# Causal scores of linear attention on TensorE: products of 64 by 128 tiles split into 64 by 64 tiles, without the covered quadrant

## The reference, cut to what matters

```python
gamma = 1.0 - 2.0 ** (-5.0 - np.arange(H, dtype=np.float32))
scale = 1.0 / np.sqrt(D)
for t in range(S):
    state = gamma[None, :, None, None] * state + np.einsum('bhd,bhe->bhde', k[:, :, t], v[:, :, t])
    y[:, :, t] = scale * np.einsum('bhd,bhde->bhe', q[:, :, t], state)
...
x = np.ascontiguousarray(attn_out.transpose(0, 2, 1, 3)).reshape(B * S, H * D)
x = _moe_ref(x=x, **moe_kwargs)
return _moe2_ref(x=x, **moe2_kwargs)
```

## Time and profile before

| what | value |
| --- | --- |
| median of 3 runs | 537.28 us |
| lowest and highest | 535.38 and 537.73 us |
| the profiled execution, its own time | 538.69 us |
| its span, first to last instruction | 536.8 us |
| mean granted TensorE clock | 0.975 |
| TensorE busy | 495.5 us, 92% of the span |
| VectorE, ScalarE, GpSimd busy | 280.7, 183.0, 255.1 us |
| moved by transfers | 106.87 MB, mean 199 GB/s |

### The profile page before, as it was taken

One profiled execution on the slowest core, in us unless ns is written; L12 is line 12 of the kernel. 1 busy time (PEld: TensorE's weight loads), 2 busy tenths in 40 slices (PEclk: granted clock), 3 DMA queues, 4 the chain that ended last, 5 costly groups with the idle time before them and its releaser, 6 DMA issues.

```text
span 536.8 us, 13517 instructions
## 1 busy us (share of the span) xinstructions
PE 495.5 (92%) x4820; PEld 288.6 (54%) x4821; DVE 280.7 (52%) x467; ACT 183.0 (34%) x322; POOL 255.1 (48%) x217
## 2 busy tenths in 40 slices
PE   4999999987985777899999999999999999999995
PEld 4877777863475343444544545445445445455452
DVE  2785777676230798563646464564645333423422
ACT  0111212221002546845555463645542222223210
POOL 1222222202000013476777868787868666666553
PEclk9998999997999789999999999999999999999998
DMA  8999999998999999343366332132332432433410
GB/s 281 398 352 387 360 384 403 382 342 319 374 426 429 405 414 387 130 164 122 159 218 200 122 119 59 21 53 42 50 53 44 55 45 44 57 43 45 58 19 0
DMA packets 35095, 106.87 MB, mean 199 GB/s; under 512 B 11871, under 2 KB 13135, under 8 KB 32624
## 3 DMA queue, kind: packets, MB, share of 16 engines
q1 hardware_dynamic: 20880, 91.85, 44.4%
q0 software_dynamic: 14176, 14.49, 15.0%
HBM read 92.82 MB, written 29.43 MB: 228 GB/s over the span
## 4 chain that ended last, share of the span: by engine, by line
PE 82%; DVE 6%; issue 5%; DMA 4%; POOL 1%; ACT 1%; SPq 0%; DVEq 0%; POOLq 0%
PE ps L1017 52%; PE ps L1000 5%; PE ps L675 4%; PE ps L739 4%; DMA late_w1a<-chunks 3%; PE ps L859 3%; PE ps L888 3%; PE ps L715 2%; PE ps L729 2%; PE ps L750 2%; PE ps L689 1%; PE ps L771 1%; DMA w_region<-chunks 1%; POOL rec_region L613 1%; PE ps L704 1%
## 5 line engine op out<-in xcount | busy, mean ns | idle before, releaser
L1017 PE MATMUL ps<-w_region,s_region 128*128 (+1 forms) x1304 | 290.4, 379 | 0.3 <-issue 0.3
L1017 PEld LDWEIGHTS ps<-w_region,s_region 128*128 128x128 f16 x1304 | 125.3, 98 | 141.6 <-issue 0.8
L1673 DVE SCALAR_TENSOR_TENSOR s_region<-ps,s_region 128x1024 f16<-128x1024 f32 x55 | 67.3, 1224 | 142.4 <-ACT s_region L1219 129.6
L1219 ACT ACTIVATE s_region<-ps 128x1024 f16<-128x1024 f32 x55 | 56.3, 1023 | 178.5 <-PE ps L1000 125.7
L619 POOL DMA_INDIRECT out<-s_region,rec_region x41 | 54.8, 1336 | 43.3 <-DVE s_region L1706 39.9
L625 POOL DMA_INDIRECT out<-s_region,rec_region x42 | 67.0, 1594 | 17.2 <-issue 11.9
L613 POOL DMA_INDIRECT rec_region<-records,idx x55 | 59.9, 1089 | 24.4 <-issue 16.3
L559 POOL TENSOR_TENSOR s_region<-w_region,s_region 128x512 f32<-128x512 f32 x14 | 14.6, 1042 | 50.8 <-PE ps L750 36.2
L1000 PEld LDWEIGHTS ps<-s_region,sw_region 128*128 (+1 forms) x440 | 29.6, 98 | 15.2 <-issue 1.9
L1706 DVE TENSOR_SCALAR s_region<-ps,rec_region,y_scale 128x512 f32<-128x512 f32 x42 | 33.8, 805 | 7.6 <-PE ps L1017 4.1
L1000 PE MATMUL ps<-s_region,sw_region 128*128 128x128 f16 x440 | 34.4, 219 | 1.6 <-issue 1.4
(11 more groups left out here) (249 smaller groups left out, 568.4 us busy)
## 6 DMA issues: line engine op xcount, KB each, us to landing
w_region<-moe_w SPq DMA_DIRECT2D x49, 512.0 KB, 9.3
w_region<-moe_w SPq DMA_DIRECT2D x10, 2048.0 KB, 10.6
w_region<-chunks SPq DMA_DIRECT2D x24, 512.0 KB, 7.2
s_region<-moe_w SPq DMA_DIRECT2D x4, 2048.0 KB, 13.6
sw_region<-chunks SPq DMA_DIRECT2D x10, 512.0 KB, 6.7
late_w1a<-chunks SPq DMA_DIRECT2D x8, 512.0 KB, 7.2
w_region<-moe_w SPq DMA_DIRECT2D x3, 1024.0 KB, 7.2
s_region<-moe_w SPq DMA_DIRECT2D x5, 512.0 KB, 8.5
```

The costliest lines, as they stand in the source:

```text
L1017: last = nc.tensor.matmul(bank[6 + r], h[:, r, f, :], w2b_parts[:, bass.ds(o, 1), part, f, :].rearrange("p e m -> p (e m)"), start=(first ...
L1219: nc.scalar.activation(h_hi[:, r, :, :].rearrange("p c t -> p (c t)").rearrange("p (a n) -> p a n", a=2), ps[:, 2 + 2 * r:4 + 2 * r, :], A ...
L1673: nc.vector.scalar_tensor_tensor(out=h_lo[:, r, :, :].rearrange("p c t -> p (c t)").rearrange("p (a n) -> p a n", a=2), in0=ps[:, 2 + 2 * ...
```

## The change

From the third chunk on (g of 2 and more) a head's product of 128 keys by 128 queries becomes two. The first takes the keys 0 to 63 and all 128 queries, the second the keys 64 to 127 and the queries 64 to 127 only. Queries 0 to 63 see none of the keys 64 to 127, so that quadrant of 64 by 64 is not computed. The mask is unchanged and still reads the whole bank: the quadrant holds what the first two chunks, which are computed in full, left in the four banks, and it is multiplied by 0. A chunk then has 16 products, in tiles of 64 by 64, in the order half, then head, inside a pair.

```diff
--- before.py
+++ after.py
@@ -672,8 +672,17 @@
                 for n in range(NP):
                     for i in range(2):
                         rows = slice(i * D, (i + 1) * D)
-                        last = nc.tensor.matmul(bank[SC[c % 2][i]][:, n * P:(n + 1) * P], kt_in[g % KV_DEPTH][rows, n, :],
-                                                qt_in[g % QK_DEPTH][rows, n, :], start=True, stop=True)
+                        if g < 2:
+                            last = nc.tensor.matmul(bank[SC[c % 2][i]][:, n * P:(n + 1) * P], kt_in[g % KV_DEPTH][rows, n, :],
+                                                    qt_in[g % QK_DEPTH][rows, n, :], start=True, stop=True)
+                    if g >= 2:
+
+                        for half in range(2):
+                            for i in range(2):
+                                rows, seen = slice(i * D, (i + 1) * D), slice(half * D, P)
+                                last = nc.tensor.matmul(bank[SC[c % 2][i]][half * D:(half + 1) * D, n * P + half * D:(n + 1) * P],
+                                                        kt_in[g % KV_DEPTH][rows, n, half * D:(half + 1) * D],
+                                                        qt_in[g % QK_DEPTH][rows, n, seen], start=True, stop=True)
                 last.then_inc(scores_ready, 1)
 
             def logit_parts_of(t):
```

## The result

The changed kernel takes **540.99 us** (median of 10 runs, 538.1 to 546.35), the kernel before 537.51 (10 runs beside it, 534.66 to 540.2). The ratio is **1.0068, 95% interval 1.0045 to 1.0092**: 3.5 us slower by the medians, beyond the 0.5% that I called "same", and 1 us above my range.

What follows compares the result with a forecast made beforehand. Stage one was taken as bounded by TensorE and, close by, the transfer engines; 8 chunks x 0.06 us = 0.5 us off the median 537.28 gave 536.8 us, range 534.9 to 540.0.

Steps and rivals of the forecast that it cites:

- same: Whole kernel: a change under 0.5%, that is 2.7 us, either way; chance 0.78.
- The burst: Scores of one chunk (L675): 1.03 us instead of 1.09, as 0.17 + 8 x 0.108.
- rival 1: Scores: tiles with unequal columns do not overlap, 0.40 us more per chunk, 544.0 us in all; chance 0.12.
- rival 4: Scores: weight loads no longer covered by products, burst near 1.95 us, 554.1 us in all; chance 0.02.
- The waits for loads take up what is saved ahead of them: Before g = 8 and 16: savings become longer load waits, so only 8 of 22 chunks count, 0.5 us.
- I expect no new limit of issue: Scores: issue doubles to 27 ns per record without a limit, since L888 keeps 192 records going at 28 ns apiece.
- The other engines' and SyncE's instructions are the same and cost nothing more: Outside TensorE: the instructions stay unchanged, so no time is added.
- their chance of 0.14: Whole kernel slower by over 0.5%, above 540.0 us, through rival 1, rival 4 or a slower chip; chance 0.14.
- The prediction's own last sign of being wrong: Whole kernel: wrong in its frame if the time moves over 2.7 us with the scores' burst at 1.03 us.

Runs made afterwards that it cites:

- after_again: The changed kernel run once more, unaltered, for a second profile; 540.06 us, ratio 1.0076 to the kernel before.
- after_light: The changed kernel with 28 of the 30 early quarters of `w1a` not loaded; 533.15 us, ratio 0.9951 to the kernel before.
- quarters: The changed kernel with split scores in four quarters of 32 array columns, all 128 queries; 571.50 us, ratio 1.0638 to the kernel before.
- split_full: The changed kernel with both halves streaming all 128 queries, nothing left out; 539.44 us, ratio 1.0035 to the kernel before.
- tiny16_light: The kernel before plus 16 unread small float16 products per chunk, with 28 of 30 early `w1a` quarters not loaded; 540.01 us, ratio 1.0059.

## Why the prediction was wrong

- **The burst** (1.03 us, 0.06 less): right. 1.02 measured; tiles with unequal columns overlap, so rival 1 was wrong, and the loads of weights stay covered, so rival 4 was too. The Trainium skill's sentence against it ("TensorE: Matmul & The Clock Gate", "The mechanism"), that a weight load overlaps running products only where the row group differs, does not hold for these tiles: by the estimate in the prediction the burst would have been near 1.95.
- **The waits for loads take up what is saved ahead of them**: not seen. They should have grown by some 0.4 us each; they shrank from 1.5 us (2.1 in the profile that I had) to 0.6 us. I put that down to TensorE coming late by itself.
- **"I expect no new limit of issue"**: this is the step that failed. I had L888 keep 192 records going for 5.45 us and took this as proof of the rate. With their weight loads these are 384 instructions, only one and a half blocks. Right behind them the same trace had three pauses of 1.38, 2.50 and 2.23 us, named "issue" and 256 records apart, and I took none of them into account. The doubled number of instructions was checked against the array's pace, not against how the instructions get there. In its place the runs showed pauses at the ends of blocks of instructions (3.1 of the 3.3 us of "issue" in stage one of `after_again`), and no cost of the split that shows where the transfer engines had less to do.
- **"The other engines' and SyncE's instructions are the same and cost nothing more"**: true, and beside the point. The queue that carries the instructions had three packets more, in a stretch where the transfer engines were full. The term missing in the sum: 22 chunks x 32 instructions = 704, 2.75 blocks. From 12 to 112 us TensorE used 13 blocks before, 15.5 after the change with its pauses, and 16.0 where nothing held it back (after_light). The kernel before gave a block 7.7 us; the split, unhindered, would give it 6.3. The way of a block beside full transfer engines, some 6 us and at times 7, had been below the one and lies around the other.
- The sign of rivals 1 and 4 was right, and their chance of 0.14 too small, for a reason that was not among them. The prediction's own last sign of being wrong came true: the time moved by more than 2.7 us with the burst at its forecast, so something outside the scores had moved. That something is the supply of instructions.

The page "Runtime: NRT & Kernel Launch" of the Trainium skill, in the section "Instruction fetch mechanics", says that instructions are refilled in blocks of 16 KiB, 256 instructions, and that the cost of crossing from one to the next is mostly hidden. The first agrees with the 256 records above. The second does not hold for the changed kernel: in stage one the cost is hidden at 7.7 us per block, and it is not at 6.5 with the transfer engines full.

## What to carry to other kernels

Splitting a product into smaller tiles buys array time and pays with instructions; before doing it, count TensorE's instructions (weight loads too, twice for float32) per microsecond in that stage, and see how full the transfer engines are. With full transfer engines next to nothing showed at one block of 256 per 7.7 us on average, there were pauses at one per 7.0, and the loss was larger than any gain of the split. With the transfer engines at 0.78 there were none at one per 6.3. Waits named "issue" that lie 256 records apart are this limit, and whether they cost depends on who waits for TensorE there: curing them at L888 gained nothing.

## What the hardware showed that was not expected

- After every pause at a block's end TensorE went on 1.2 to 1.6 us after the block's packet; in `quarters`, for one, a packet lay between 81.0 and 82.2, and TensorE went on at 83.58. So over a microsecond passes between landing and use, beyond the wait for the transfer engines.
- After a pause for instructions of 2.86 us the granted clock was 0.72 from 42 to 48 us, so part of that stretch was at 1.2 instead of 2.4 GHz (`quarters`). In `after_again`, where no pause in stage one was longer than 1.25 us, it stayed at 1.00.
- Tiles of 64 by 64 with 128 and with 64 columns in one burst cost nearly as much as with 128 columns in all: the burst takes 1.02 to 1.03 us here and 1.03 to 1.04 (64.76 to 65.80, 60.02 to 61.05) in `split_full`. That what a tile leaves out would be won if its neighbours left it out too was not tried.
- Still open: how much of the loss beyond stage one (3.5 to 4.4 us in all, 2.6 at the mark in one pair of profiles) comes from the later blocks' new borders (the pauses at L888 are 6.1 and 3.8 us in the two profiles before, 5.5 in `after_again`), and why tiny16_light lost more than its tiny products.
